# The first gram waits for the identity alone, two engines issue the first keys, and TensorE multiplies the identity with itself while it waits

## The reference, cut to what matters

```python
k_n = k / (norm(k) + 1e-6)
for t in range(768):                       # per batch and head, state is 48 x 48
    y[t]  = q[t] @ state
    state = state + beta[t] * outer(k_n[t], v[t] - k_n[t] @ state)
x = y.reshape(3072, 384)
h = x @ w_in                               # 384 -> 2048
x = where(h >= 1, h, where(h <= -1, 0, (h + 1)**2 / 4)) @ w_out
xn = x / rms(x) * rms_g
y = (silu(xn @ w_gate) * (xn @ w_val)) @ w_out2
```

## Time and profile before

| | us |
|---|---|
| median of 3 runs | 1074.31 |
| lowest, highest of the runs | 1073.03, 1076.67 |
| the profiled execution | 1073.82 |
| its span, first to last instruction | 1072.0 |
| TensorE matmul, VectorE, ScalarE, GpSimd busy | 1041.4, 580.2, 427.9, 9.6 |

### The profile page before, as it was taken

The page is one execution under the profiler, slowest core; times in us unless marked ns, Lnnn a source line. Parts: engine busy times, 40 slices in busy tenths (PEclk is TensorE's granted clock), DMA queues, the critical chain, the costliest instruction groups (busy, mean ns, idle before and its releaser), DMA issues.

```text
span 1072.0 us, 24895 instructions
## 1 busy us (share of the span) xinstructions
PE 1041.4 (97%) x11116; PEld 861.0 (80%) x11116; DVE 580.2 (54%) x1017; ACT 427.9 (40%) x728; POOL 9.6 (1%) x20
## 2 busy tenths in 40 slices
PE   6999999999999999999999999999999999999996
PEld 3589888777777777777778888888888888888885
DVE  5978769858947848863356435324324234333322
ACT  5745534443454454353476543132232232232211
POOL 1000000000000000000000000000000000000000
PEclk9999999999999999999999999999999999999999
DMA  8604004102300410030030230200200200100101
GB/s 245 173 4 118 3 4 124 26 4 61 89 3 3 119 31 3 31 120 2 2 119 30 89 118 1 59 1 1 60 1 2 59 1 1 30 1 1 30 1 29
DMA packets 19033, 48.08 MB, mean 45 GB/s; under 512 B 2448, under 2 KB 9232, under 8 KB 17872
## 3 DMA queue, kind: packets, MB, share of 16 engines
q1 hardware_dynamic: 18928, 46.51, 15.7%
HBM read 37.06 MB, written 9.44 MB: 43 GB/s over the span
## 4 chain that ended last, share of the span: by engine, by line
PE 80%; DVE 12%; issue 3%; ACT 2%; DMA 2%; SPq 0%; DVEq 0%; ACTq 0%
PE bank L690 21%; PE hps L1235 14%; PE acc L1250 13%; PE acc L709 10%; PE hps L690 7%; PE hps L709 4%; DVE outer L992 3%; DVE inv L996 2%; DVE g L1065 2%; PE acc L1268 2%; DVE g1l L1073 2%; PE bank L1194 1%; PE bank L1180 1%; PE bank L1173 1%; DVE tt L1006 1%
## 5 line engine op out<-in xcount | busy, mean ns | idle before, releaser
L607 ACT ACTIVATE g<-bank 128x512 f32<-128x512 f32 x72 | 43.1, 599 | 257.2 <-PE bank L690 142.6
L1235 PE MATMUL hps<-xh,w1h 128*128 128x512 f32 (+1 forms) x336 | 129.9, 387 | 4.0 <-DVE g L1065 3.0
L895 ACT ACTIVATE g1h<-g 128x512 fp32r<-128x512 f32 (+1 forms) x112 | 63.9, 571 | 169.4 <-DVE g L1065 144.6
L1250 PE MATMUL acc<-g1h,w2h 128*128 128x512 f32 (+1 forms) x336 | 127.7, 380 | 1.7 <-DVE g1l L1073 1.4
L1235 PE MATMUL hps<-xh,w1l 128*128 128x512 f32 (+1 forms) x336 | 122.0, 363 | 0.0
L1250 PE MATMUL acc<-g1h,w2l 128*128 128x512 f32 (+1 forms) x336 | 122.0, 363 | 0.0
L1235 PE MATMUL hps<-xl,w1h 128*128 128x512 f32 (+1 forms) x336 | 121.9, 363 | 0.0
L1250 PE MATMUL acc<-g1l,w2h 128*128 128x512 f32 (+1 forms) x336 | 121.8, 363 | 0.0
L1073 DVE TENSOR_TENSOR g1l<-g,g1h 128x512 fp32r<-128x512 f32 (+1 forms) x112 | 68.6, 613 | 71.0 <-ACT g1h L895 70.4
L1065 DVE SCALAR_TENSOR_TENSOR g<-hps,g 128x512 f32<-128x512 f32 (+1 forms) x112 | 68.1, 608 | 50.9 <-ACT g L889 50.5
L886 ACT ACTIVATE g<-hps,half_c 128x512 f32<-128x512 f32 (+1 forms) x112 | 69.7, 622 | 55.7 <-PE hps L1235 55.6
(11 more groups left out here) (173 smaller groups left out, 2044.4 us busy)
## 6 DMA issues: line engine op xcount, KB each, us to landing
kqT<-kq SPq DMA_DIRECT2D x22, 384.0 KB, 6.4
v_in<-v SPq DMA_DIRECT2D x6, 768.0 KB, 4.6
k_in<-k SPq DMA_DIRECT2D x6, 768.0 KB, 5.5
x2d<-x2s SPq DMA_DIRECT2D x18, 256.0 KB, 5.5
x2t<-x2d SPq DMA_DIRECT2D x6, 768.0 KB, 5.9
y<-y_t SPq DMA_DIRECT2D x48, 96.0 KB, 2.2
stage<-w_in SPq DMA_DIRECT2D x4, 768.0 KB, 8.3
stage<-w_out SPq DMA_DIRECT2D x4, 768.0 KB, 8.7
```

The costliest lines, as they stand in the source:

```text
L607: act.activation(silu[:, f % 2, :], gps[f % 2][:, :], ACT.Silu).then_inc(e_silu, 1)
L895: act.activation(g1h[:, f % 2, 0:WIDTH[n]], g1[:, f % 2, 0:WIDTH[n]], ACT.Copy).then_inc(s_gh, 1)
L1235: last = pe.matmul(hps[f % 2][:, 0:WIDTH[n]], wt[:, kk, P * f:P * f + P], xx[:, kk, COLS[n]], start=(kk == 0 and e == 0), stop=(kk == KD - ...
L1250: last = pe.matmul(acc[j][:, 0:WIDTH[n]], wt[:, f, P * j:P * j + P], gg[:, f % 2, 0:WIDTH[n]], start=(f == 0 and e == 0), stop=(f == NF1 - ...
```

## The change

The list of chunk 0 begins with 7 multiplications of the identity with itself on TensorE (128x128, fp32, into a PSUM bank that piece 2 overwrites), and 12 more follow GK. The four key DMAs are split: SP issues both halves of bp 0, ScalarE both halves of bp 1, each the first half first. TensorE waits for the identity alone (s_const 1), ScalarE for the first four constants (identity, two masks, 0.5). ScalarE's wait for all 8 stands now before nrm of chunk 0.

```diff
-    out = [("GK", 0, hf) for hf in range(HALVES)]
+    out = [("warm", 0, 7), ("GK", 0, 0), ("GK", 0, 1), ("warm", 0, 12)]
...
+            def first_keys(eng, bp):
+
+                eng.dma_start(kqT[0][C * bp:C * bp + D, 0, 0:NPAIR, :].rearrange("p i t -> p (i t)"),
+                              kq[0, 0, bp, :, 0:NPAIR * C]).then_inc(s_k0, 16)
+                eng.dma_start(kqT[0][C * bp:C * bp + D, 0, NPAIR:NINST, :].rearrange("p i t -> p (i t)"),
+                              kq[0, 0, bp, :, NPAIR * C:NINST * C]).then_inc(s_kq[0][0], 16)
...
-                    for bp in range(BP):
-                        sp.dma_start(kqT[0][C * bp:C * bp + D, 0, 0:NPAIR, :].rearrange("p i t -> p (i t)"),
-                                     kq[0, 0, bp, :, 0:NPAIR * C]).then_inc(s_k0, 16)
-                    for bp in range(BP):
-                        sp.dma_start(kqT[0][C * bp:C * bp + D, 0, NPAIR:NINST, :].rearrange("p i t -> p (i t)"),
-                                     kq[0, 0, bp, :, NPAIR * C:NINST * C]).then_inc(s_kq[0][0], 16)
+                    first_keys(sp, 0)
                     sp.dma_start(beta_i[:, :, :].rearrange("p c t -> p (c t)"), beta[:, :]).then_inc(s_beta, 16)
...
                         elif kind == "nrm":
+                            if c == 0:
+                                act.wait_ge(s_const, N_CONST)
...
-                    act.wait_ge(s_const, N_CONST)
+                    first_keys(act, 1)
+                    act.wait_ge(s_const, 1 + MEM + 1)
                     act.activation(rnrm[:, 0:1], half_c[:, 0:1], ACT.Sqrt).then_inc(s_neg, 1)
...
                     def split(u):
                         kind, _, p = u
+                        if kind == "warm":
+                            for _ in range(p):
+                                pe.matmul(acc[2][:, 0:P], ident[:, :], ident[:, :], start=True, stop=True)
...
-                    pe.wait_ge(s_const, N_CONST)
+                    pe.wait_ge(s_const, 1)
```

## The result

| | us |
|---|---|
| after, median of 20 runs | 1076.47 (1073.54 to 1082.11) |
| before, median of 20 runs beside them | 1074.34 (1073.00 to 1076.74) |
| ratio, 95% interval | 1.0022 [1.0012, 1.0031] |
| the profiled execution after | 1077.51, span 1075.6 |

The change costs 2.1 us between the medians, and the ratio of the runs is 1.0022. My forecast was 1073.6 and its range ended at 1075.9; the sign of the expected 0.5 us was wrong too.

The account below looks back on a forecast made before the run. Before 57.2 us two chains, TensorE's and VectorE's, were taken to set U. VectorE's 0.5 us, the smaller gain, turned 1073.82 into 1073.3, or 1073.8 as median; forecast 1073.6, range 1071.7 to 1075.9.

Parts of the forecast that it names:

- the expected 0.5 us: Forecast gain at the kernel's end: the smaller of VectorE's 0.5 us and TensorE's 1 to 3.5 us.
- hide in the wait for keys: Before the first gram: seven fillers take 3.3 us, 1.6 to 4.9, while TensorE waits for keys anyway.
- both chains: TensorE's and VectorE's sequences of work before the first network, said to meet at U within 0.03 us.
- late keys: Rival: table load precedes ScalarE's key issues, last key lands about 7.5, everything behind 0.4 us later; 1074.5, chance 0.10.
- idle fillers: Rival: fillers don't raise the clock level, piece 0 starts 0.9 us later, TensorE sets U; 1075.0, chance 0.10.
- TensorE's chain: Pieces through Z and X to U: pieces 0 to 2 take 3.3 instead of 6.3 us; chain up 1 to 3.5.
- somewhat less at U because of the later weight chunks: Allowance on TensorE's 3 us gain from faster pieces, for weight chunks landing later; no size given.
- VectorE's chain: Transposes, nrm, then 34.3 us to scaled v, which U needs; hangs on weight chunk 1, moves up 0.5 us.
- a queue that moves up 0.5 as a whole: SP's queue behind the last key: everything 0.5 us earlier, weight chunk 1 from 15.2 to 14.7.
- Key transfers: First four key DMAs, split over two queues: first gram from about 4.9, last key landing 0.5 us earlier.
- the lower bound: Least gain at the last key's landing: none, as all four transfers pass at the same rate; upper bound 0.91 us.
- The rival that two queues double the rate: Keys overlap at up to twice the rate, landing up to 1.9 us earlier; nrm gains 1.2 to 1.5; 1072.6, chance 0.15.

Follow-up runs that it names:

- e9: Kernel before plus only 19 multiplications of 32x32 at the fillers' places (38 pairs); ratio to before 1.0015 [1.0005, 1.0025].
- e6: Changed kernel with its 19 fillers shrunk to 32x32, same 38 pairs; ratio to before 1.0023 [1.0009, 1.0037].
- e5: Changed kernel with fillers four times as wide, 2 and 3 instead of 7 and 12 (10 pairs); ratio to before 0.9993 [0.9981, 1.0005].
- e1: Changed kernel without its 19 fillers, split keys and early waits kept; ratio to before 1.0000 [0.9992, 1.0009].
- e11: Changed kernel with nrm of chunk 0 ahead of hi 1 and only 3 wide fillers, behind the grams; ratio to before 0.9987, run again 0.9996.
- e14: Kernel before with only weight chunk 6 issued ahead of the q keys of chunk 0; ratio to before 1.0004 [0.9992, 1.0015].
- e5b: Second measurement of the changed kernel with wide fillers, 2 and 3; ratio to before 1.0001 [0.9989, 1.0014].
- e8: Changed kernel with wide fillers (2 and 3) and nrm of chunk 0 moved ahead of hi 1; ratio to before 0.9995 [0.9986, 1.0003].
- e2: Changed kernel with all four key transfers issued by SP as before, fillers and early waits kept; ratio to before 1.0023 [1.0009, 1.0038].
- e4: Changed kernel with only the 12 fillers behind the second gram (24 pairs); ratio to before 1.0003 [0.9991, 1.0014].
- e12: Kernel before plus only 44 multiplications of 32x32 at the fillers' places (88 pairs); ratio to before 1.0028 [1.0015, 1.0041].
- e3: Changed kernel with only the 7 fillers ahead of the first gram (14 pairs); ratio to before 1.0020 [1.0010, 1.0031].

## Why the prediction was wrong

**The step that failed** is the one in which the fillers "hide in the wait for keys" and cost nothing else. I counted their time and never their instructions. Each is two loads and two multiplications, the block end moves ahead by as many pairs, and in U it stands in the one step for which both chains wait. What the runs showed in its place: 38 pairs with next to no work cost 0.15% (e9) to 0.23% (e6), 1.6 to 2.5 us; nearly the same work in 10 pairs (e5), or no fillers (e1), cost nothing. The sign for it was in the trace of before, the stop of 0.30 us in GQ, and I had not read it. No rival of mine had it either: the slower ones were late keys (1074.5, the last key was in fact 0.1 us early) and idle fillers (1075.0, they did raise the level).

**TensorE's chain "up by 1 to 3.5"** was wrong as well. hi 5 starts 1.86 us earlier (29.66 for 31.52), hi 6 0.26 later (37.18 for 36.92), and of the gain 0.47 us are left at Z (44.96 for 45.43). Z and X then lose them: Z takes 0.19 us longer, and X, cut by the stop of 0.23 us, 0.43 (2.64 for 2.21), so that X ends 0.15 late. Chunk 6 is what I had waved through with "somewhat less at U because of the later weight chunks". In the profiled executions other than e11's hi 6 starts between 35.22 (e14) and 38.36 us (e5b), and the same kernel has 36.07 in e5 and 38.36 in e5b, so the kernels' parts do not set it alone. ScalarE's copy of X, TensorE's side, still releases U, and VectorE's 0.88 us are worth nothing.

**VectorE's chain** was read rightly, and its size was luck. It gained 0.85 us at nrm, not 0.5, since weight chunk 1 landed 0.85 earlier; but the reason that I gave, a queue that moves up 0.5 as a whole, is not in the trace: the last key came 0.1 us earlier, chunk 0 landed 0.54 later (12.32 for 11.78), and no run shows what set chunk 1. The rest of the chain went as said: hi 1 cut the transposes' 1.55 us down to the 0.85 (VectorE idle 1.20 us before nrm), and e8 confirms it with 1.15 more.

**Key transfers.** The gain is 0.1 us, next to the lower bound, where I took 0.5: the transfers, not the queue, set the landing. The second of the two that the first gram needs even landed later than before, at 5.24 for 4.99, so that gram starts at 5.29 and not at 4.9. The rival that two queues double the rate falls (6.99 against 5.2). The Trainium skill, "DMA: Bandwidth & Descriptors", section "Issuing engines are not separate DMA queues", by which issuing from several engines saves only the time of the issue, gave the better value here. The ACT_TABLE_LOAD stands behind the two new issues, at 1.65 instead of 0.73, so the rival of late keys falls too. That is where the Trainium skill, "ScalarE: Activation LUTs", section "Step-by-step: what each stage is for", has it.

**The granted level.** That it rises before the pieces was right for the grams and wrong for the pieces: TensorE was idle for 2.85 us before piece 0 and the level fell at its second multiplication. Nor do fillers of either kind give the level for certain. In e2, with the same 19, both grams took 1.99 us. With wide fillers e5 waited 1.13 us ahead of the pieces and kept the level (1.02 us for two), e8 waited 3.15 and kept it, e5b waited 2.11 and lost it (1.91 us for two from the second piece). The length of the wait alone does not decide it.

**How much is the stop and how much the level** stays partly open. In the profiled execution of e6 the gap is 0.61 us, the level stays high, and the network starts at 57.5, only 0.3 later than before. Of e6's twelve executions the three with a mean granted clock of 0.998, the profiled one among them, took 1074.6 to 1075.4 us, as the kernel before does; the nine with 0.990 to 0.997 took 1077.1 to 1079.9. On average e6 has 0.9945, e1 0.9985, and the runs of before beside e6 0.9970. So most of the loss comes in executions in which the level falls, as in the change's own profile (1.92 of 3.67 us lie behind U's end, and a part of U's 1.61 is of the level). That the stops make the fall likelier is what these averages suggest, not what they show. In e2 and e9 the level falls within the gap of U, in e4 and e12 behind a gap; in the change's profile it falls at about 52.3 us, 0.2 ahead of the gap in U and behind the one in X; in e3 and e6 it does not fall there at all.

## What to carry to other kernels

An added instruction that fills an idle engine costs more than its time if it moves the end of a block of instructions onto the critical chain, as the 38 pairs did here: count the instructions between two blocks, and look for a long run of small ones on the critical chain. Do filling with few wide instructions, not many small ones (10 pairs cost nothing here). And when two chains meet within 0.1 us, an early start of either is worth nothing until both are followed to their next wait.

## What the runs showed of the hardware that I had not expected

TensorE stops at a fixed count of instructions. From stop to stop are 124 to 127 pairs of weight load and multiplication (124 in e1 from GQ to Z, 126 and 127 in e8), so 248 to 254 instructions; the rest, I take it, are waits that the records leave out. The stops in Z, X and U are 0.15 to 1.2 us long.

The instruction queue shows the blocks themselves. The profile of before has 87 transfers on it with 1.43 MB, 16.4 KB each, and TensorE's 22232 recorded instructions make 87 blocks of 256. Beside each stop is one: cut into quarters of a microsecond, the DMA tables have it from 50.75 us in the change, from 50.0 in e4, 53.75 in e9 and 46.75 in e12, and TensorE goes on 2.2 to 2.8 us later. In e8 the two are at 45.75 and 49.75, each about 0.9 us behind a restart and 2.8 to 3.0 ahead of the next: together the 3.8 to 3.9 us that a block took there, however short its work.

The Trainium skill, "Runtime: NRT & Kernel Launch", section "Instruction fetch mechanics", says that instructions are refilled in blocks of 16 KiB, 256 instructions, and that crossing into a block costs little and is mostly hidden. The first agrees with the counts and with the 0.02 MB of each transfer in the instruction queue. The second does not hold in these runs of 64 small multiplications; the measurement decides.
